# Sharing the last sixteen keys' transpose between two pairs of heads, and moving the attention steps by a slot

## The reference

```python
k_p = k.reshape(B, H, 72, 8, D).mean(axis=3)
v_p = v.reshape(B, H, 72, 8, D).mean(axis=3)
scores = scale * np.matmul(q, k_p.transpose(0, 1, 3, 2))
attn = softmax(scores)                       # over the 72 keys
x = np.matmul(attn, v_p)                     # -> [4608, 512]
h = x @ moe_w_in                             # 512 -> 2048
g = 0 if h <= -1 else h if h >= 1 else (h + 1) ** 2 / 4
y = g @ moe_w_out                            # 2048 -> 512
out = maximum(y @ moe2_w_in, 0) ** 2 @ moe2_w_out
```

## Time and profile before

| | |
|---|---|
| time, median of 3 runs | 1576.3 us (1575.58 to 1576.34) |
| the profiled execution | 1576.08 us, of which its span is 1574.3 us |
| PE busy | 1565.2 us (99% of the span) |
| DVE, ACT, POOL busy | 1146.3, 861.7, 247.8 us |
| granted TensorE clock | 1.0 in the whole span |
| slots with attention (72.8 to 484 us) | 26% of the span |

### The profile page before, as it was taken

The page is one execution under the profiler, slowest core; times in us unless marked ns, Lnnn a source line. Parts: engine busy times, 40 slices in busy tenths (PEclk is TensorE's granted clock), DMA queues, the critical chain, the costliest instruction groups (busy, mean ns, idle before and its releaser), DMA issues.

```text
span 1574.3 us, 25577 instructions
## 1 busy us (share of the span) xinstructions
PE 1565.2 (99%) x9173; PEld 1548.1 (98%) x9173; DVE 1146.3 (73%) x1883; ACT 861.7 (55%) x1608; POOL 247.8 (16%) x356
## 2 busy tenths in 40 slices
PE   8999999999999999999999999999999999999999
PEld 6999999999999999999999999999999999999999
DVE  7777667677666867877879777666667986876874
ACT  5777678767676644444445654444456643443442
POOL 7645338725500000000000000000000000000000
PEclk9999999999999999999999999999999999999999
DMA  8366469557537544344244642442448645245231
GB/s 286 105 225 229 172 208 327 188 198 231 187 123 231 170 161 142 100 161 146 96 161 153 235 146 96 161 151 103 148 157 290 194 150 192 80 140 186 91 116 41
DMA packets 173951, 262.80 MB, mean 167 GB/s; under 512 B 16640, under 2 KB 153856, under 8 KB 173824
## 3 DMA queue, kind: packets, MB, share of 16 engines
q1 hardware_dynamic: 173824, 261.16, 49.7%
HBM read 154.14 MB, written 106.95 MB: 166 GB/s over the span
## 4 chain that ended last, share of the span: by engine, by line
PE 95%; DVE 2%; ACT 1%; issue 1%; DMA 0%; POOL 0%; DVEq 0%; POOLq 0%; ACTq 0%
PE bank L854 42%; PE bank L726 25%; PE bank L877 22%; PE bank L686 2%; PE bank L697 1%; DVE gf L1290 1%; DVE b L1283 1%; PE bank L716 1%; PE bank L718 1%; PE bank L717 1%; PE bank L715 1%; DVE f_lo L1258 0%; PE bank L701 0%; DMA k_raw<-k 0%; ACT pT_rest L931 0%
## 5 line engine op out<-in xcount | busy, mean ns | idle before, releaser
L854 PE MATMUL bank<-gf,f_hi 128*128 128x384 f32 x2688 | 682.6, 334 | 0.5 <-DVE u_b L1300 0.4
L854 PEld LDWEIGHTS bank<-gf,f_hi 128*128 128x128 f32 x2688 | 485.3, 188 | 1.3 <-DVE u_b L1300 0.9
L854 PE MATMUL bank<-gf,f_lo 128*128 128x384 f32 x1344 | 448.9, 334 | 0.0
L990 ACT ACTIVATE gf<-b 128x768 fp32r<-128x768 f32 x336 | 278.5, 845 | 263.1 <-PE bank L854 174.1
L1290 DVE TENSOR_TENSOR gf<-b,gf 128x768 fp32r<-128x768 f32 x336 | 314.4, 951 | 43.4 <-ACT gf L990 43.4
L877 PE MATMUL bank<-xf,w_hi 128*128 128x384 f32 x1344 | 340.8, 334 | 0.0
L726 PE MATMUL bank<-x_hi,wi_hi 128*128 128x384 f32 x752 | 260.1, 346 | 0.5 <-DVE g_st L1371 0.5
L854 PEld LDWEIGHTS bank<-gf,f_lo 128*128 128x128 f32 x1344 | 252.3, 188 | 0.0
L726 PE MATMUL bank<-x_hi,wi_lo 128*128 128x384 f32 x752 | 252.2, 335 | 0.0
L726 PE MATMUL bank<-x_lo,wi_hi 128*128 128x384 f32 x752 | 252.2, 335 | 0.0
L877 PEld LDWEIGHTS bank<-xf,w_hi 128*128 128x128 f32 x1344 | 242.4, 188 | 0.0
(11 more groups left out here) (103 smaller groups left out, 1499.7 us busy)
## 6 DMA issues: line engine op xcount, KB each, us to landing
b<-g_dram SPq DMA_DIRECT2D x192, 384.0 KB, 4.1
g_dram<-g_st SPq DMA_DIRECT2D x192, 192.0 KB, 2.3
g_dram<-c_st SPq DMA_DIRECT2D x192, 192.0 KB, 1.9
s_dram<-su_s SPq DMA_DIRECT2D x24, 512.0 KB, 2.9
k_raw<-k SPq DMA_DIRECT2D x32, 288.0 KB, 3.5
q_sb<-q SPq DMA_DIRECT2D x48, 192.0 KB, 2.8
y_dram<-o_st SPq DMA_DIRECT2D x48, 192.0 KB, 1.9
x_raw<-y_dram SPq DMA_DIRECT2D x24, 384.0 KB, 5.4
```

Source lines behind the costliest of these rows:

```text
L854: last = mm(dst[:, 0:H], w[:, 2 * i + kt, cols], x[:, half, kt, :], start=q_ < 3 and i == 0 and kt == 0 and h == 0, stop=q_ >= 4 and i == ...
L990: copy(gf[layer][r % GRING][:, 0], unit_source(n)[:, 2 * i:2 * i + 2, :], ACT.Copy).then_inc(gf_hi, 1)
```

## The change

For pairs from 8 on, an even pair and the odd one behind it put their last 16 keys' probabilities side by side into one `rest` tile of 32 columns for each token tile (`rest_at`). Only the odd pair transposes it and copies it to `pT_rest` (32 rows instead of 16), and the even pair's `values` waits for the odd pair's `p_ready`. The last values' rows are loaded to the upper or the lower 16 rows of each 32, by the parity of the pair; the other rows are zero. Steps 0 to 4 of all these pairs stand one slot earlier. `values` and `tokens` of an odd pair stay where they were (slots 4a - 15 and 4a - 14), and those of an even pair stand three slots later than before (4a - 12 and 4a - 11).

```diff
         def rest_rows(a):
             if a < REST_APART:
-                return [(tr_ps[0:REST, 0:H], slice(0, H))]
-            return [(tr_ps[32 * t:32 * t + REST, 0:P], slice(t * P, (t + 1) * P)) for t in range(NT)]
+                return [(tr_ps[0:rest_keys(a), 0:H], slice(0, H))]
+            return [(tr_ps[32 * t:32 * t + 32, 0:P], slice(t * P, (t + 1) * P)) for t in range(NT) if a % 2]
+        def rest_keys(a):
+            return REST * (a % 2 + 1)
+        def rest_at(a):
+            return a % 2 if a < REST_APART else a // 2 % 2
...
         def pairs_at(g, step):
             first = {4: 1, 5: 4, 6: 7, 7: 9}
-            return [a for a in range(HP, PAIRS) if first.get(a, 4 * (a - 5)) + step == g
-                    and (a > HP or step > 2)]
+            def taken_at(a):
+                if a < REST_APART:
+                    return first[a] + step
+                return 4 * (a - 5) - 1 + step + (step > 4) * (1 if a % 2 else 4)
+            return [a for a in range(HP, PAIRS) if taken_at(a) == g and (a > HP or step > 2)]
...
                 for row in range(0, REST_ROWS, 32):
-                    sp.dma_start(v_raw[n][row:row + REST, 1], v_rest[m // HP, m % HP]).then_inc(v_in[n], 16)
+                    first = row + REST * n
+                    sp.dma_start(v_raw[n][first:first + REST, 1], v_rest[m // HP, m % HP]).then_inc(v_in[n], 16)
...
                     if a < REST_APART:
-                        last = tr(tr_ps[0:REST, cols], probs[:, t, MAIN:KEYS], ident[:, :])
-                if a >= REST_APART:
-                    last = tr(tr_ps[0:32 * NT, 0:P], rest[a % 2][:, :, :], ident[:, :])
+                        n = rest_keys(a)
+                        last = tr(tr_ps[0:n, cols], probs[:, t, KEYS - n:KEYS], ident[:, :])
+                if a >= REST_APART and a % 2:
+                    last = tr(tr_ps[0:32 * NT, 0:P], rest[rest_at(a)][:, :, :], ident[:, :])
...
             def values(a):
-                pe.wait_ge(p_ready, a + 1)
+                pe.wait_ge(p_ready, a + 1 if a < REST_APART or a % 2 else a + 2)
                 pe.wait_ge(v_ready, keys_of(a))
                 if a > HP:
                     pe.wait_ge(x_ready, a)
```

More of the change, by code:

```diff
@@ L710, in values @@
                     pe.wait_ge(x_first_ready, a)
-                hi, lo, rows = pT_hi[a % 2], pT_lo[a % 2], pT_rest[a % 2]
+                hi, lo, rows = pT_hi[a % 2], pT_lo[a % 2], pT_rest[rest_at(a)]
                 last = None
@@ L927, in probabilities @@
                     act.wait_ge(pv_full, a - 1)
-                copy(pT_hi[a % 2][:, :], tm_ps[:, 0:H], ACT.Copy)
+                last = copy(pT_hi[a % 2][:, :], tm_ps[:, 0:H], ACT.Copy)
                 for row in (0, 64):
                     for src, dst in rest_rows(a):
-                        last = copy(pT_rest[a % 2][row:row + REST, dst], src, ACT.Copy)
+                        last = copy(pT_rest[rest_at(a)][row:row + src.shape[0], dst], src, ACT.Copy)
                 last.then_inc(p_hi_ready, 1)
@@ L1227, in normal @@
                     second = share[a % 2].rearrange("p (t h) -> p t h", h=2)[:, :, 1:2]
-                    vec.tensor_tensor(rest[a % 2][:, :, 0:REST], prob[a % 2][:, :, MAIN:KEYS],
+                    first = REST * (a % 2)
+                    vec.tensor_tensor(rest[rest_at(a)][:, :, first:first + REST], prob[a % 2][:, :, MAIN:KEYS],
                                       second.broadcast_to([P, NT, REST]), ALU.mult).then_inc(s_rest, 1)
@@ L1235, in probabilities_low @@
                 dve.wait_ge(p_hi_ready, a + 1)
-                vec.tensor_tensor(pT_lo[a % 2][:, :], tm_ps[:, 0:H], pT_hi[a % 2][:, :].bitcast(F32), ALU.subtract)
+                last = vec.tensor_tensor(pT_lo[a % 2][:, :], tm_ps[:, 0:H], pT_hi[a % 2][:, :].bitcast(F32),
+                                         ALU.subtract)
                 for src, dst in rest_rows(a):
-                    rows = pT_rest[a % 2]
-                    last = vec.tensor_tensor(rows[32:32 + REST, dst], src, rows[0:REST, dst].bitcast(F32), ALU.subtract)
+                    rows, n = pT_rest[rest_at(a)], src.shape[0]
+                    last = vec.tensor_tensor(rows[32:32 + n, dst], src, rows[0:n, dst].bitcast(F32), ALU.subtract)
                 last.then_inc(p_ready, 1)
@@ L1423, in _ @@
             normal(4)
-            for one in rest:
-                vec.memset(one[:, :, REST:], 0.0)
             for g in range(-4, SLOTS):
```

## The result

| | before | changed |
|---|---|---|
| time, median of 6 runs each | 1576.37 us | 1584.8 us (1584.28 to 1587.12) |
| ratio, 95% interval | | 1.0055 (1.0044 to 1.0065) |
| profiled execution | 1576.08 us | 1585.24 us |
| its span | 1574.3 us | 1583.4 us |

A forecast was written before the change was run, and what follows sets the result against it. PE was taken to bound the kernel, busy without waits during attention. 1576.08 - 2.2 (transposes) + 7.1 (late x_lo) + 1.2 (start) = 1582.2 us profiled, plus 0.2 to the median: 1582.4 us; range 1577.2 to 1586.0 us.

The forecast's parts named there:

- The transposes, -2.2 us: On PE, 20 of the 40 last-keys transposes go, at 0.11 us each: 2.2 us saved.
- The rival with 273 ns a piece: A transpose costs PE its whole 273 ns record and no chain is late: 1570.8 us, chance 0.05.
- The hidden edits: Fewer ACT copies and DVE subtractions, 32-row copies, moved loads, and even values waiting for odd low parts: 0 us.
- The late `x_lo`, +7.1 us: PE's odd values wait for the even pair's x_lo, later still where keys pooling precedes it on DVE: +7.1 us.
- the six that were forecast to lose 0.76 us: Odd pairs 11, 13, 23, 25, 35, 37: pooling in slot, one set of values, uncut next score; 0.76 us each.
- the three at 0.40: Odd pairs 15, 27, 39: pooling in their slot and a next score cut in four; 0.40 us each.
- the three at 0.22: Odd pairs 17, 29, 41: pooling in their slot and themselves cut; 0.22 us each.
- those at 0.15: Odd pairs 9, 21, 33, 45: the short wait for x_lo without the pooling; 0.15 us each.
- The start, +1.2 us: Pair 8's earlier steps delay pair 7's copies and values, then pair 8's transposes stall near 70 us: +1.2 us.
- The rival with a chance of 0.02: PE's clock halves for one slot behind each of the 16 short waits: 1616 us, chance 0.02.
- the sum's own range: The bounds of the summed terms, from 1579.4 to 1584.8 us.
- the delay that spreads: Rival: the next pair's transposes also wait behind late x_lo, 12 x 0.4 us more: 1587 us, chance 0.12.

The follow-up runs named there:

- doubled ones: The kernel before with each of the 40 last-keys transposes made twice into the same place: 1580.3 us, ratio 1.0026.
- the second profile of the changed kernel: The changed kernel timed and profiled once more, with only a comment line added at its top: 1583.99 us, ratio 1.0051.
- the earlier steps alone: The kernel before with only steps 0 to 4 of pairs from 8 on one slot earlier, nothing shared: 1578.97 us, ratio 1.0018.

## Why the prediction was right, and where it was off

**What bounds the kernel** held: PE, and only what PE does or waits for. ACT and DVE gave up 47 us between them for nothing.

**The transposes, -2.2 us.** Measured at 0.10 us each with doubled ones, 2.1 us for 20. The rival with 273 ns a piece is out.

**The hidden edits.** 32 rows cost a copy what 16 did (265 ns both, x120 after, x240 before); the new wait of `values(even)` for the odd pair's low parts shows only at `values(46)`, which starts at 489.85, 0.05 us behind the end of L1259; before, `values(47)` waited for L1239 in the same way, so nothing is lost by it.

```profile
L949 ACT ACTIVATE pT_rest<-bank 32x128 fp32r<-32x128 f32 x120 | 31.8, 265 | 1.2
```

**The late `x_lo`, +7.1 us.** The mechanism and the places were right: first `values(odd)` one slot behind `values(even)`, then the pooling in the same slot, three heights of wait (by starts, 0.9, 0.5 and 0.3 us). The size was 8.5 us in the profiled run. The first product of slot 174 starts 9.11 us later than before, and 2.66 of it stood there already at slot 16 (72.82 in the earlier trace rows, then 76.12, less the 0.64 of pair 9's scores, which now stand ahead of that point); the 20 transposes are 2.1 less. The rows are the start of slot 174 before, and of slots 16 and 174 after:

```profile
484.35 0.34 PE L726 MATMUL bank<-x_hi,wi_hi 128*128 128x384 f32 x1
76.12 0.44 PE L744 MATMUL bank<-x_hi,wi_hi 128*128 128x384 f32 x1
493.46 0.34 PE L744 MATMUL bank<-x_hi,wi_hi 128*128 128x384 f32 x1
```

By pairs, read from starts in the same way: the six that were forecast to lose 0.76 us lost 0.86 to 0.91, the three at 0.40 lost 0.45 to 0.57, the three at 0.22 lost 0.33, and those at 0.15 about 0.16 to 0.19. Of the 13 to 16 waits that the profile was to show, nine do; the others are hidden by the overlap of the records. Two terms of a single wait were too small. The pooling was taken at 0.68 us, by the overlap of neighbours; it took 0.78, from 107.84 to 108.62. And a wait that ends was taken at 0.06 + 0.11 us; here it was 0.15 from the end of `x_lo` at 111.91 to 112.06, and 0.08 more for the next product. 0.76 + 0.10 + 0.06 is the 0.92 us measured.

**The start, +1.2 us.** `values(7)` was forecast to go on as from 69.67 and started at 69.68, and the transposes of pair 8 as from 71.51 (71.43). By slot 16 the loss without a dip of the clock is 74.38 - 72.82 - 0.64 = 0.9 us in the second profile of the changed kernel. In the first it is 2.66 us.

**The clock.** The rival with a chance of 0.02 came true in part. It fell not with the 16 short waits but once, behind the two stalls of the start, for 3 us, and the difference of the two profiles by slot 16 is 2.66 - 0.92 = 1.7 us. The rule that was set beside it (Trainium skill, "TensorE: Matmul & The Clock Gate", A second HAM failure mode: psum-queue depth-cycling) is about a clock that swings because PE idles for short times between groups of matmuls often enough; by that rule the waits further on could have brought the clock down again. This trace shows no such swing: with nine waits of 0.3 to 0.7 us, the clock is 1.00 from 90 to 484 us.

```profile
90.00:484.00 394.00, 388.79 (x2358) 378.79 (x2357) 254.18 (x564) 255.74 (x558) 190.87 (x276) 1.00 0.62 204
```

So 1582.4 us missed the median by 2.4 us: 1.4 us in the size of the waits, and for the rest the profiles show two things that vary from run to run, the clock at the start and the late stores around slots 82 to 93. How much of the rest is which in the runs without a profile stays open. The median of 1584.8 us is the upper end of the sum's own range. The room above it, to 1586.0, was for the delay that spreads, and that didn't come: in the first profile PE has no idle time for `prob` behind the start. Open as well is why the earlier steps alone cost 2.7 us in the median: about 1 us is the start's, its profiled execution lost 0.8 by late stores and more by the low clock, but 9 of the 11 executions had a mean clock of 1.000 and took as long.

## What to carry to other kernels

An engine that was never waited for can have no slack at all: before the change nobody needed `x_lo` at that moment, and the timeline already showed it ending 0.02 us ahead of the point where somebody would. When steps of a hand-written order move by a slot, list for each moved wait what now stands between producer and consumer, and what stands in the same queue ahead of the producer, here a pooling that had been in an idle place. If one slot is too short, giving the consumer a second one (here one digit) was worth far more than the work saved.

## What the hardware showed unexpectedly

- The two stalls near 70 us leave PE busy for 1.2 and 1.4 us of two stretches of 2 us. Behind them the granted clock fell to the lower of its two levels, 1.2 GHz (0.57 and 0.50 in the window from 72 to 74 us), in two of the five profiled executions that have them. Over all executions of the changed kernel, of the experiments and of the kernel before beside them, the mean clock was 0.999 in 9 of the 44 of kernels with these stalls, and 1.000 in all 86 of kernels without them.
- In slots 76 to 93, while the next product's weights are loaded, ACT's longest wait for the store of a `g_st` buffer was 0.28 us in one profile of the changed kernel and 1.51 us in the other, and 2.31 us with the earlier steps alone. A chain without slack passes it on to PE. Why a store lands so late isn't shown.
- A wait of PE that has ended costs 0.17 to 0.23 us beyond the end of what it waited for: 0.06 to 0.15 to the start, and 0.08 to 0.11 more for the next product, since the weights were not loaded ahead of the wait.
